# Weight residues of the last stage moved from VectorE to GpSimd, with reordered loads and splits around the change of stage

## What is computed

```
u = x + h.transpose(0, 2, 1)
h2 = np.maximum(u @ w_ch1, 0.0) @ w_ch2      # 512 -> 1536 -> 512, 4608 tokens
return u + h2
```

## Time and profile before

| | |
|---|---|
| median of 3 executions | 1214.44 us |
| the profiled execution | 1213.61 us, its span 1211.8 us |
| PE, share of the span busy | 98% |
| DVE / ACT / POOL | 69% / 40% / 28% |
| mean granted clock of TensorE | 0.995 |
| last instruction of POOL's list | in stage C; it is idle in all of stage D |

### The profile page before, as it was taken

How to read it: one execution, slowest core, us unless ns; L and a number is a source line. 1 busy time by engine, 2 the same in 40 slices (tenths; PEclk the granted TensorE clock), 3 DMA queues, 4 the chain that set the end, 5 groups by cost and what they waited for, 6 DMA issues and landing times.

```text
span 1211.8 us, 20530 instructions
## 1 busy us (share of the span) xinstructions
PE 1182.7 (98%) x7590; PEld 1150.9 (95%) x7590; DVE 836.4 (69%) x1227; ACT 490.0 (40%) x764; POOL 338.2 (28%) x209
## 2 busy tenths in 40 slices
PE   6999999999999999999999899999999999999998
PEld 5899999999999999999898899999999899999998
DVE  3877778686868778678556566766766786666664
ACT  3532424242433324244433455555556543333331
POOL 4443534444252525440553042133210000000000
PEclk9999999999999999999999999999999999999999
DMA  9825445272543440036998587856669999989973
GB/s 254 172 53 112 79 94 101 39 156 39 111 76 86 78 107 10 34 87 227 344 300 295 164 332 267 298 201 263 248 233 334 382 304 300 271 240 308 290 189 53
DMA packets 348428, 228.12 MB, mean 188 GB/s; under 512 B 268880, under 2 KB 316368, under 8 KB 347344
## 3 DMA queue, kind: packets, MB, share of 16 engines
q1 hardware_dynamic: 348368, 227.32, 64.7%
HBM read 136.84 MB, written 92.80 MB: 189 GB/s over the span
## 4 chain that ended last, share of the span: by engine, by line
PE 91%; DMA 3%; DVE 2%; issue 1%; ACT 1%; SPq 1%; POOL 0%; DVEq 0%; POOLq 0%; ACTq 0%
PE bank L42 11%; PE bank L44 11%; PE bank L43 11%; PE bank L1267 10%; PE bank L1269 10%; PE bank L1268 10%; PE bank L309 6%; PE bank L314 6%; PE bank L308 6%; PE bank L240 3%; PE bank L265 3%; PE bank L279 1%; PE bank L253 1%; DMA attention_g<-g_scratch 1%; DMA qkv_x_tokens<-x_tokens_scratch 1%
## 5 line engine op out<-in xcount | busy, mean ns | idle before, releaser
L308 PE MATMUL bank<-weights_tok,z_z 128*128 128x288 f32 x576 | 164.2, 299 | 0.0
L309 PE MATMUL bank<-weights_tok,z_z 128*128 128x288 f32 x576 | 161.3, 295 | 0.0
L314 PE MATMUL bank<-weights_tok,z_z 128*128 128x288 f32 x576 | 124.8, 294 | 0.0
L309 PEld LDWEIGHTS bank<-weights_tok,z_z 128*128 128x128 f32 x576 | 108.2, 188 | 0.0
L308 PEld LDWEIGHTS bank<-weights_tok,z_z 128*128 128x128 f32 x576 | 108.1, 188 | 0.0
L838 POOL TENSOR_TENSOR weights_rms_inverse<-weights_mean_squares,weights_minus_half 128x8 f32<-128x8 f32 x40 | 65.5, 1639 | 129.6 <-DVE weights_mean_squares L632 129.3
L314 PEld LDWEIGHTS bank<-weights_tok,z_z 128*128 128x128 f32 x576 | 92.6, 188 | 0.0
L519 ACT ACTIVATE weights_x_channel_major<-attention_u 128x288 fp32r<-128x288 f32 x64 | 28.4, 444 | 139.4 <-DVE attention_u L699 138.8
L853 POOL TENSOR_TENSOR z_z<-tokens_cos,z_z 128x512 fp32r<-128x512 f32 x24 | 34.5, 1437 | 173.5 <-ACT z_z L512 173.5
L42 PE MATMUL bank<-weights_x_channel_major,weights_ch 128*128 128x288 f32 x256 | 77.2, 301 | 0.0
L43 PE MATMUL bank<-weights_x_channel_major,weights_ch 128*128 128x288 f32 x256 | 75.4, 294 | 0.0
(11 more groups left out here) (287 smaller groups left out, 3697.7 us busy)
## 6 DMA issues: line engine op xcount, KB each, us to landing
g_scratch<-attention_staged SPq DMA_DIRECT2D x36, 960.0 KB, 5.0
weights_g<-g_scratch SPq DMA_DIRECT2D x24, 1152.0 KB, 10.3
g_scratch<-attention_staged SPq DMA_DIRECT2D x36, 384.0 KB, 5.6
x_scratch<-attention_u SPq DMA_DIRECT2D x8, 1152.0 KB, 4.5
u_scratch<-attention_u SPq DMA_DIRECT2D x8, 1152.0 KB, 6.2
weights_raw_u<-u_scratch SPq DMA_DIRECT2D x6, 1536.0 KB, 7.4
qkv_u_left<-u_scratch SPq DMA_DIRECT2D x12, 768.0 KB, 9.4
qkv_k<-in_k_dram SPq DMA_DIRECT2D x32, 256.0 KB, 4.9
```

Of the source, the lines that this page charges most:

```text
L308: pe.matmul(out, x, wtok[0][:, zt, hs], start=(i == 0), stop=False)
L309: pe.matmul(out, x, wtok[1][:, zt, hs], start=False, stop=False)
L314: mm = pe.matmul(tok_bank(b, g)[:, 0:HALF], z[1][:, zt, c * P:(c + 1) * P], wtok[0][:, zt, half * HALF:(half + 1) * HALF], start=False, st ...
```

## The change

1. The residues of the seven weights are subtracted on POOL, in a list of its own at the end of its program, and no longer on DVE. The subtraction is the same, as is its operand size, 1536 elements in each of 128 partitions. PE waits for POOL's semaphore in place of DVE's.
2. On SPq's list, the load of SECOND's operand stands before `store_late(34)` and `load_u2(0, 0)`, behind the weight of THIRD.
3. On ACT's list, `hi` of SHARED stands before unit 35's copy to `bank_f` and its ReLU of tile THIRD, and no longer behind them.
4. On DVE's list of stage D, in each group, the split `lo` of the next group's FIRST stands before `seed_e(0)` and `c22(0)`.
5. On SPq's list of stage C, `w2_load(0)` and `w2_copy` stand ahead of everything, where before they were at units 1 and 3.

```diff
     def sync(sp, nxt):                      # phase_c
         sp.wait_ge(*prev["p_y"])
+        w2_load(sp, 0)
+        w2_copy(sp)
         for n in range(UNITS):
             g, i = divmod(n, NI)
             if i == 1 and g + 1 < NG:
                 load(sp, g + 1)
-            if n == 1:
-                w2_load(sp, 0)
-            if n == 3:
-                w2_copy(sp)
...
+            if n == UNITS:
+                nxt["hi"](act, 0, SHARED)
             if 1 <= n <= UNITS:
                 act.wait_ge(p[LATE], n)
                 wait(act, a_g21, n - 1)
                 act.activation(bank_f, bank_a(n - 1), ACT.Copy).then_inc(a_f, 1)
                 relu(n - 1, THIRD, tile(n - 1, THIRD), (d_c22, n), a_g22)
-            if n == UNITS:
-                nxt["hi"](act, 0, SHARED)
...
-                if n == UNITS - 3:
-                    nxt["weight_lo"](dve, FIRST)
...
-    def weight_lo(dve, k):
-        dve.wait_ge(a_w, k + 1)
-        dve.tensor_tensor(weight(k, 1), weight(k, 1).bitcast(F32), weight(k, 0).bitcast(F32),
-                          ALU.subtract).then_inc(d_w, 1)
+    def gpsimd(gp):
+        for k in range(NP):
+            gp.wait_ge(a_w, k + 1)
+            gp.tensor_tensor(weight(k, 1), weight(k, 1).bitcast(F32), weight(k, 0).bitcast(F32),
+                             ALU.subtract).then_inc(g_w, 1)
...
         elif step == 5:
             sp.wait_ge(last, UNITS - 3)
             load_operand(sp, 0, MIDDLE)
             load_weight(sp, THIRD)
+            sp.wait_ge(last, UNITS - 2)
+            load_operand(sp, 0, SECOND)
         elif step == 6:
             sp.wait_ge(prev["p"][MIDDLE], UNITS)
             sp.wait_ge(prev["d_c22"], UNITS)
             load_u2(sp, 0, 0)
-            sp.wait_ge(last, UNITS - 2)
-            load_operand(sp, 0, SECOND)
...
             out12(g, 0)
             out12(g, 1)
+            split(M + 7)
             seed_e(g, 0)
             c22(g, 0)
-            split(M + 7)
             seed_e(g, 1)
```

More of the change, by code:

```diff
@@ L1585, in vector @@
                         prep_lo(dve, g + 1, k)
-                if n == UNITS - 3:
-                    nxt["weight_lo"](dve, FIRST)
                 if n == UNITS - 2:
                     nxt["lo"](dve, 0, FIRST)
-                if n == UNITS - 1:
-                    nxt["weight_lo"](dve, SHARED)
             if n == UNITS:
                 nxt["lo"](dve, 0, SHARED)
-                nxt["weight_lo"](dve, MIDDLE)
     def gpsimd(gp, nxt):
@@ L1632, in phase_d @@
     a_hi, d_lo = sem("d_act_ghi"), sem("d_dve_glo")
-    a_w, d_w = sem("d_act_whi"), sem("d_dve_wlo")
+    a_w, g_w = sem("d_act_whi"), sem("d_pool_wlo")
     d_b, d_t12, d_t22, d_c, d_e, d_c22, d_x = [sem(f"d_dve_{x}") for x in (
@@ L1767, in product @@
             if g == 0:
-                pe.wait_ge(d_w, k + 1)
+                pe.wait_ge(g_w, k + 1)
         for t in range(FT):
@@ L1889, in vector @@
             seed_b(g, 1)
-            if g == 0:
-                weight_lo(dve, SECOND)
             split(M + 3)
@@ L1894, in vector @@
             take12(g, 1)
-            if g == 0:
-                weight_lo(dve, THIRD)
             split(M + 4)
@@ L1899, in vector @@
             seed_c(g, 1)
-            if g == 0:
-                weight_lo(dve, LATE)
             split(M + 5)
@@ L1906, in vector @@
             out11(g, 1)
-            if g == 0:
-                weight_lo(dve, LAST)
             split(M + 6)
@@ L1921, in vector @@
         out21(NG - 1, 1)
-    return dict(sync=sync, tensor=tensor, scalar=scalar, vector=vector,
-                ahead=ahead, weight_hi=weight_hi, weight_lo=weight_lo, hi=hi, lo=lo, first=first)
+    return dict(sync=sync, tensor=tensor, scalar=scalar, vector=vector, gpsimd=gpsimd,
+                ahead=ahead, weight_hi=weight_hi, hi=hi, lo=lo, first=first)
 def region(ctx, nc, name, size, *users):
@@ L2072, in _ @@
             c["gpsimd"](eng, d)
+            d["gpsimd"](eng)
 _INS = ['q', 'k', 'v', 'g_norm', 'moe_w_theta', 'moe_w_tok_r', 'moe_w_tok_i', 'moe_w_ch',
```

## The result

| | before | changed |
|---|---|---|
| median, side by side (5 and 5 executions) | 1215.75 us | 1224.67 us |
| the profiled execution, its span | 1213.61, 1211.8 us | 1224.31, 1222.2 us |

The ratio is 1.0068, 95% interval 1.0047 to 1.0091: the change makes the kernel slower, by 8 us (5.7 to 11 us). The forecast was 1219.2 us with a range up to 1222. The direction was right, the size was not, and the time lies outside the range.

What follows compares the result with a forecast made beforehand. PE, busy 98% of the span, was taken as the bound, so only its gaps and clock count. LAST's delay +3.5 and the clock +1.7 made +5.2 us, forecast 1219.2 us, 8-in-10 range 1212.5 to 1222.

Steps and rivals of the forecast that it cites:

- the term of the early `w_ch2` traffic: Stage C's start: 3.9 MB go ahead of group 1's raw input; cost 0, ends 0 and +1.5 us.
- a rival with 8%: Stage C's start: what ACT lacks while idle queues behind 10 us of DMA traffic; half as delay, +5, 1224 us; 8%.
- Moving the residues: Change of stage: each of POOL's seven subtractions can hold a DVE split by up to 3.5 us.
- the split ahead of `seed_e`: Before LAST, first group: FIRST's next split, 2.5 us, delays the seed; PE starts LAST +3.5 us, ends 0.8 and 3.7.
- The clock: At LAST: PE's clock falls after a 4.0 us wait, +1.7 us, ends 0 and 1.7.
- SECOND first: Stage D loads: SECOND lands 3.1 us earlier, `seed_b` and MIDDLE may start 1 to 3 us late; cost 0.
- `hi` of SHARED first: On ACT: 2.1 us go ahead of the copy to `bank_f`, which PE needs only after FIRST's matmuls; cost 0.
- Landing follows issue: Before THIRD: its load, issued earlier, lands as much earlier, up to 3.9 us gained, 1210.5 us; 10%.
- the working by the bytes: Before THIRD: the bytes ahead are the same and the queue refills 1.4 us later, so loads land 1.2 us later.
- No exclusion that matters: Change of stage: splits and POOL's instructions miss each other, LAST starts 0.8 us late, clock stays, 1215.2 us; 25%.

Runs made afterwards that it cites:

- b_w2early: The kernel before with only the loads and copies of `w_ch2` moved to the start of stage C; ratio to before 1.0027.
- b_w2one: The kernel before with one of the four `w_ch2` loads (384 KB) early, the other three and the copies where they were; ratio to before 1.0029.
- a_nosplit: The changed kernel without the early `w_ch2` traffic and without the next group's FIRST split ahead of `seed_e`; ratio to before 1.0017.
- b_poolbut: The kernel before with six of the seven residues on POOL, that of LAST's weight staying on DVE; ratio to before 1.0008.
- b_hold: The kernel before with the last store of `u` (1152 KB) held until ACT has made the copy of THIRD; ratio to before 0.9977.
- b_order: The kernel before with the two reorderings alone: SECOND's operand loaded earlier, and `hi` of SHARED earlier on ACT; ratio to before 0.9999.

## Why the prediction was wrong, and where it was right

- **The step that failed is the term of the early `w_ch2` traffic, "Cost 0, ends 0 and +1.5".** Measured: +4.6 us by the traces, 2.3 of them PE's longer gap behind ACT's idle time and 2.3 the clock; with this part alone (b_w2early) +4.7 us, by the ratio 0.27%. The working followed the bytes to the data that they delay (the load of `u`, which ACT indeed took at 699.78 without a wait), and did not follow them to ACT's idle time, 2.96 us "issue" that nothing explained. That idle time was made a rival with 8%, and the rival came true. That traffic ahead of it lengthens it is shown; that it is made of late instructions is inferred. Its price of 5 us came close to 4.6 by luck: it took half of 10 us of traffic as delay, while the idle time grew by 2.3 us, nearly all of it from the first 384 KB (b_w2one), and the clock made up the rest.
- **Moving the residues, the split ahead of `seed_e`: right.** A split waits for POOL's subtraction as in the earlier trace rows (3.95 and 3.96 us in place of 2.56), LAST came 3.5 us late as forecast (PE's longest gap was the one at stage C's start, though, and not this one), and a_nosplit and b_poolbut take the two contributions away one by one. That the end stretch agrees to the tenth, +5.24 and +5.2, is in part luck: the profile of before holds a fall of the clock at THIRD that costs 1.2 us, and against the 290.2 of b_hold, which has no fall there, the changed kernel's end is 6.5 us longer.
- **The clock: right at LAST** (1.7 us), and missed at stage C's start, since no longer gap was forecast there. That it did not fall after 2.3 us in the earlier trace rows was one of two outcomes, as the other profiles show.
- **SECOND first and `hi` of SHARED first: 0, right** (b_order 0.9999), and for SECOND by the reason given: PE waited 1.9 us for the first seed, and THIRD had no gap any more. The two were not tried apart.
- **The other rivals.** "Landing follows issue" supposed that THIRD's load is issued earlier. It was issued at 957.29, which is 4.2 us later than before counted from the mark, and ACT had it 43.3 us behind the mark in place of 42.1: 1.2 us later, as the working by the bytes had it, and not 4.2. "No exclusion that matters" fell with the 3.96 us.
- With the failed step's 4.6 us the sum is 9.8, and 1213.61 + 9.8 = 1223.4 for the profiled 1224.31; 0.6 of the rest lie ahead of stage C.

## What to carry over

An engine's idle time for which the profile names no releaser is a row to be tested, not left: here one small edit, a store held back for a few microseconds, showed what it hung on and was worth more than the change. When bulk transfers are moved earlier, look not only at the data that they delay but at every such idle time in the stretch into which they move; here it ended each time 1.2 to 1.9 us behind a packet of the instruction queue. And before two delays at one gate are added, subtract the gate's slack once: two edits that alone left gaps of 0.8 and 1.2 us before LAST made one of 3.6 together, and only behind that one the clock fell. Last, when stretches of single profiles are compared, see first whether the clock fell in both.

## Not expected of the hardware

- ACT's idle time without a releaser at the start of stage C: 0.87 us with idle DMA engines, 2.96 behind a store of 1152 KB, 5.04 with one load of 384 KB more, and no more than 5.29 with ten times as much.
- PE's clock fell after a gap of 2.3 to 2.4 us in 5 of 9 profiles, for the same instructions and the same gap; a single trace does not settle whether it will.
